# Attention by pairs of heads, with tiled matmuls, ahead of and inside a two-layer MLP kernel on one core

## The chip, the core and the metric

The kernel runs on one core of a Trainium2 chip. A core has TensorE (PE in the profile), which multiplies from SBUF into PSUM, VectorE (DVE), ScalarE (ACT) and GpSimd (POOL), each with its own instruction queue worked in order, and a sync engine (SP) that issues DMAs. The metric is the device time of one execution in microseconds (us).

## What is computed

A banded attention with four sink keys (2 batches, 8 heads, 768 positions, head size 64), then a squared-ReLU MLP, then an MLP with a rational activation, both 512 to 2048 to 512 over 1536 tokens, all in fp32:

```python
scores = scale * np.matmul(q, k.transpose(0, 1, 3, 2))
keep = is_sink | in_window            # n_sink = 4, window = 128
scores = np.where(keep, scores, -1000000000.0)
a = np.exp(scores - np.max(scores, axis=-1, keepdims=True))
a = a / (np.sum(a, axis=-1, keepdims=True) + 1e-09)
x = np.matmul(a, v)                   # to (1536, 512)
h = np.maximum(x @ w_in, 0.0)
x = h * h @ w_out
h = x @ w_in2
g = (a0 + a1*h + a2*h**2 + a3*h**3) / (1 + |b0| |h| + |b1| h**2 + 1e-6)
return g @ w_out2
```

## The kernel before

The 1536 tokens form 12 query tiles of 128 (`TILES`), three to a block (`QT`), four blocks (`BLOCKS`). Queries of tile i look at the keys of their own and the previous tile and at 32 sink columns (`SINK_CAP`), so a head's scores are 128 x 288 (`BAND`), 128 x 128 in the first tile of a batch and 128 x 256 in its second.

**Attention** goes head by head. A *unit* u is one head of one query tile, 96 in all (`U_ALL`). In a slot s each engine does its part of several units: TensorE scores unit s (`score`, L1196 or L1200), turns the probabilities of unit s-2 (`turn_p`, L1216, L1218 for the sinks of four heads at once) and weighs the values for unit s-3 (`weigh`, L1233, L1240 for sinks). VectorE adds the mask and takes the row's minimum of the negated scores (L925), ScalarE takes the exponential with its row sum (L656); the turned probabilities are copied from PSUM to `bpT` by VectorE for even units (L935) and by ScalarE for odd ones (L647). In the first 32 units (`k < EARLY`) a score is one fp32 matmul; TensorE works an fp32 matmul as two records in the trace. Later ones are two fp32r matmuls (L1200, one record each), for which GpSimd splits queries and keys into a high and a low part (`split_kq`, L468 to L488); the input is packed with each head's 64 features twice, so that the contraction is over 128 rows. In `weigh` the turned probabilities are the stationary operand (128 x 128) and 64 columns of values move; the output has queries on rows. After a tile's eighth head VectorE divides by the row sums (`finish`, L941 to L949, into `o_sb`), TensorE transposes the result (`tile_out`, L1259), and ScalarE and VectorE write it as a high and a low part into `xT` (L672, L966).

**The lead.** The first 30 slots (`LEAD`) run with nothing else on TensorE. Scores and turned probabilities have a bank each, and in the lead a second of each (`score_bank`, `turn_bank`): `s_ps` for even units, `y_ps` for odd ones. So `score(u)` waits only until VectorE has read the scores of unit u-2.

**The steady part.** The other slots lie inside the first MLP (layer 1). Per step i a block needs `first` (L1146, 12 matmuls of 384 columns) and `second1` (L1158, 12 more); a list (`events`) puts one slot or tile output after each half of 12 matmuls: after the second group of three in `first` and after the second in `second1`. Between them ScalarE and VectorE square the hidden values (L594, L842, L599, L848). Blocks 0 to 2 carry attention this way; block 3 and the second MLP (L1384 and on) carry none.

## Time and profile before

| | us |
|---|---|
| median of 3 runs | 672.12 (670.58 to 672.66) |
| profiled execution, its own time | 672.72 |
| its span, first to last instruction | 670.9 |
| lead: first score matmul to the first matmul of layer 1 | 7.70 to 44.52 |
| layer 1 with attention inside | 44.52 to 320.32 |
| rest of layer 1 | 320.32 to about 392 |
| second MLP | about 392 to 670.9 |

| engine | busy us | share of the span |
|---|---|---|
| PE | 654.5 | 98% |
| PEld (weight load, overlaps PE) | 617.3 | 92% |
| DVE | 447.9 | 67% |
| ACT | 377.7 | 56% |
| POOL | 330.9 | 49% |

The records of matmuls overlap: each lasts longer than the distance to the next. What a matmul costs in a stream is the distance between starts, read from the timeline, and its record's length beyond that is the time until its result is there.

### The profile page before, as it was taken

The numbers are of one execution on the slowest core, as the hardware profiler recorded it, in microseconds if no ns is written. First come the engines' busy times: TensorE is split into PE (matmuls) and PEld (weight loads), VectorE is DVE, ScalarE is ACT, GpSimd is POOL, SyncE is SP. The second block draws the span as 40 slices with busy tenths as digits, with TensorE's granted clock in tenths as the row PEclk, the third lists the DMA queues.
The fourth block names the chain that finished last, engine by engine and source line by source line (L and its number), as shares of the span: only waits on it lengthen the run. The fifth ranks groups of instructions, "written<-read, shape, count | busy, mean of one in ns | idle before, by whom it ended". The sixth has DMA issues, their size and how long they took to land.

```text
span 670.9 us, 10181 instructions
## 1 busy us (share of the span) xinstructions
PE 654.5 (98%) x3714; PEld 617.3 (92%) x3714; DVE 447.9 (67%) x665; ACT 377.7 (56%) x804; POOL 330.9 (49%) x316
## 2 busy tenths in 40 slices
PE   7999999999999999999999998999999999999997
PEld 6889998999999999999999997889899999999995
DVE  6656564444344344343466679999899989998995
ACT  3755555334444354443322256677877787778874
POOL 3968573313242212300022337777777767776773
PEclk9999999999999999999999999999999999999999
DMA  7743241203311113100043430002100210001001
GB/s 248 258 146 119 97 162 40 64 1 121 93 40 40 40 40 134 40 9 1 20 125 124 127 110 0 1 1 95 48 1 0 95 48 0 1 1 48 1 0 53
DMA packets 28971, 43.49 MB, mean 65 GB/s; under 512 B 4080, under 2 KB 19440, under 8 KB 28400
## 3 DMA queue, kind: packets, MB, share of 16 engines
q1 hardware_dynamic: 28912, 42.74, 19.6%
q8 instruction: 32, 0.52, 0.3%
...
## 4 chain that ended last, share of the span: by engine, by line
PE 77%; DVE 14%; ACT 3%; issue 3%; POOL 2%; DMA 1%; DVEq 0%; SPq 0%; ACTq 0%; POOLq 0%
PE h_ps L1146 22%; PE y_ps L1158 18%; PE y_ps L1384 15%; PE s_ps L1146 7%; PE o_ps L1233 4%; PE o_ps L1146 3%; DVE s_ps L879 3%; PE s_ps L1216 2%; PE s_ps L1200 2%; DVE o_ps L879 2%; DVE sq L842 2%; DVE p_buf L882 1%; DVE p_buf L873 1%; DVE h_ps L879 1%; DMA y_scratch<-xT 1%
## 5 line engine op out<-in xcount | busy, mean ns | idle before, releaser
L1146 PE MATMUL h_ps<-xT,weights 128*128 128x384 f32 x960 | 190.2, 340 | 0.7 <-ACT sq L594 0.7
L1146 PEld LDWEIGHTS h_ps<-xT,weights 128*128 128x128 f32 x960 | 167.4, 188 | 2.5 <-issue 1.0
L1158 PE MATMUL y_ps<-hid,weights 128*128 128x384 f32 x768 | 156.7, 344 | 0.0
L1384 PE MATMUL y_ps<-weights,hid 128*128 128x512 f32 x576 | 144.3, 395 | 2.3 <-POOL hid L561 1.0
L1158 PEld LDWEIGHTS y_ps<-hid,weights 128*128 128x128 f32 x768 | 134.5, 188 | 0.7 <-issue 0.2
L1384 PEld LDWEIGHTS y_ps<-weights,hid 128*128 128x128 f32 x576 | 107.2, 188 | 24.3 <-POOL hid L561 2.4
L656 ACT ACTIVATE bprobs<-bnegs,neg_max 128x288 f32<-128x288 f32 (+2 forms) x96 | 72.0, 759 | 67.2 <-DVE neg_max L925 66.8
L842 DVE TENSOR_TENSOR sq<-sq 128x384 f32<-128x384 f32 x64 | 45.4, 710 | 88.9 <-ACT sq L594 88.8
L561 POOL TENSOR_TENSOR hid<-p_buf,hid 128x384 fp32r<-128x384 f32 x63 | 64.8, 1028 | 40.0 <-ACT hid L762 39.6
L552 POOL TENSOR_TENSOR q_buf<-h_abs,q_buf 128x384 f32<-128x384 f32 x64 | 64.8, 1013 | 34.5 <-ACT q_buf L617 32.0
L879 DVE RECIPROCAL s_ps<-q_buf 128x384 f32<-128x384 f32 x31 | 79.4, 2561 | 3.2
L848 DVE TENSOR_TENSOR hid<-sq,hid 128x384 fp32r<-128x384 f32 x64 | 53.4, 835 | 37.8 <-ACT hid L599 37.8
L482 POOL TENSOR_SCALAR bq_hi<-q_raw 128x512 fp32r<-128x512 f32 x16 | 10.7, 668 | 136.6 <-DMA q_raw<-in_q_pack 115.2
L458 POOL TENSOR_SCALAR weights<-weights_raw 128x1024 fp32r<-128x1024 f32 x24 | 26.2, 1092 | 104.3 <-DMA weights_raw<-in_w_pack 104.1
L594 ACT ACTIVATE sq<-h_ps 128x384 f32<-128x384 f32 x64 | 31.4, 491 | 74.6 <-PE h_ps L1146 74.6
L1146 PE MATMUL s_ps<-xT,weights 128*128 128x384 f32 x384 | 72.5, 337 | 0.0
L1146 PEld LDWEIGHTS s_ps<-xT,weights 128*128 128x128 f32 x384 | 68.3, 188 | 2.5
L556 POOL TENSOR_TENSOR p_buf<-p_buf,h_sb 128x384 f32<-128x384 f32 x64 | 65.3, 1020 | 0.0
L599 ACT ACTIVATE hid<-sq 128x384 fp32r<-128x384 f32 x64 | 33.6, 524 | 51.4 <-DVE sq L842 51.4
L925 DVE CUSTOM_DVE_ANT_0 bnegs<-s_ps,band_bias 128x288 f32<-128x288 f32 (+2 forms) x81 | 34.3, 423 | 36.2 <-PE s_ps L1200 30.3
L762 ACT ACTIVATE hid<-p_buf 128x384 fp32r<-128x384 f32 x63 | 33.0, 524 | 28.9 <-DVE p_buf L882 27.6
L617 ACT ACTIVATE q_buf<-h_abs,abs_b 128x384 f32<-128x384 f32 x64 | 45.4, 709 | 2.1
...
## 6 DMA issues: line engine op xcount, KB each, us to landing
...
```

The costliest lines, as they stand in the source:

```text
L552: pool.tensor_tensor(q_buf[:, i % RING, :], h_abs[:, i % RING, :], q_buf[:, i % RING, :], ALU.mult).then_inc(qmul_ready, 1)
L556: pool.tensor_tensor(p_buf[:, i % RING, :], p_buf[:, i % RING, :], h_sb[:, i % RING, :], ALU.mult).then_inc(pmul_ready, 1)
L561: pool.tensor_tensor(hid2[:, i % RING, LO, :], p_buf[:, i % RING, :], hid2[:, i % RING, HI, :].bitcast(F32), ALU.subtract).then_inc(hid_re ...
L617: nc.scalar.activation(q_buf[:, i % RING, :], h_abs[:, i % RING, :], ACT.Identity, scale=abs_b[:, 1:2], bias=abs_b[:, 0:1]).then_inc(lin_r ...
L656: nc.scalar.activation(bprobs[:, u // GROUP % 2, cols, m % GROUP], bnegs[:, u % N_RING, cols], ACT.Exp, scale=-1.0, bias=neg_max[:, m:m + ...
L842: nc.vector.tensor_tensor(sq[:, i % 2, :], sq[:, i % 2, :], sq[:, i % 2, :], ALU.mult).then_inc(act1_ready, 1)
L848: nc.vector.tensor_tensor(hid[:, i % 2, LO, :], sq[:, i % 2, :], hid[:, i % 2, HI, :].bitcast(F32), ALU.subtract).then_inc(hid_ready, 1)
L879: nc.vector.reciprocal(h_banks[r], q_buf[:, r, :]).then_inc(qinv_ready, 1)
L925: nc.vector.tensor_tensor_reduce(out=bnegs[:, u % N_RING, cols], in0=score_bank(u)[:, cols], in1=band_bias[:, kind, cols], scale=-SCALE, s ...
L1146: ins = nc.tensor.matmul(bank, weights[:, i, wp, W_IN, t * P:(t + 1) * P], x, start=(t == 0 and n == 0), stop=(t == KC - 1 and n == 2))
L1158: ins = nc.tensor.matmul(y_ps[:, m, 0:NT], weights[:, i, wp, W_OUT, m * P:(m + 1) * P], hid[:, i % 2, gp, :], start=(i == 0 and n == 0), s ...
L1384: ins = nc.tensor.matmul(y_bank(turn, t), hid2[:, i % RING, gp, t * P:(t + 1) * P], weights[:, i, wp, W_OUT, :], start=(i == 0 and n == 0) ...
```

## The change

Heads are worked in pairs. A pair p is heads 2c and 2c+1 of a query tile, 48 in all (`P_ALL`); `LEAD` is 15 pairs.

- **Scores.** Inputs are packed with two heads' features on rows 0 to 63 and 64 to 127. Each head's score is one fp32 matmul whose operands lie on 64 rows, one head above the other, into two banks. This holds for all pairs; the fp32r form and GpSimd's splits of queries and keys are gone.
- **Weighing.** 64 columns of values are stationary and 128 turned probabilities move; the two heads write rows 0 to 63 and 64 to 127 of the same bank, so features lie on rows. For sinks there are two matmuls of 128 moving columns in place of one of 256.
- **Division.** The reciprocal row sums are spread over 512 columns (`sums`), transposed on TensorE (`turn_inv`), copied by ScalarE (`inv_copy`) and multiplied by VectorE (`divide`); the transpose of the output goes. VectorE also packs the sinks of four heads (`pack_sinks`).
- **Banks.** One pair of banks (`pair_bank`) holds a pair's scores and then its turned probabilities. In the lead there is a second set for odd pairs. `score(p)` waits for both copies of pair p-2.
- **Order.** A step "A" scores pair p and weighs pair p-2; a step "B" turns pair p-1. In "B" ScalarE takes the second exponential of pair p and then copies for pair p-1. "M" divides, "X" and "L" write the high and low part, "F" turns the reciprocals. In the steady part "A", "B" and "F" take the places that slots had.

```diff
-    U_ALL = H * TILES
-    LEAD = 30
-    EARLY = 8
+    P_ALL = PAIRS * TILES
+    LEAD = 15
...
-        q_raw3 = sb("q_raw3", [P, 3, GROUP * P], F32, band)
-        bk_raw = sb("bk_raw", [P, H, BAND], F32, band)
-
-        bkT = sb("bkT", [P, H, BAND], F32R, band)
-        bq_hi = sb("bq_hi", [P, 2, GROUP * P], F32R, band)
-        bq_lo = sb("bq_lo", [P, 2, GROUP * P], F32R, band)
+        bq = sb("bq", [P, 3, 2 * P], F32, band)
+
+        bk = sb("bk", [P, PAIRS, BAND], F32, band)
...
-        bprobs = sb("bprobs", [P, 2, BAND, GROUP], F32, band)
-        bpT = sb("bpT", [P, P_RING, 3 * P], F32, band)
+        bprobs = sb("bprobs", [P, 2, GROUP, BAND], F32, band)
+        bsinks = sb("bsinks", [P, 2, GROUP, SINK_CAP], F32, band)
+        bpT = sb("bpT", [P, P_RING, 2, 3 * P], F32, band)
...
+        inv_rows = sb("inv_rows", [P, H, D], F32, band)
+        inv_cols = sb("inv_cols", [P, DM], F32, band)
+        x_sb = sb("x_sb", [P, DM], F32, band)
...
+        def pair_bank(p, hp):
+            return y_ps[:, hp, :] if p < LEAD and p % 2 else s_ps[:, hp, :]
+
+        def wait_turned_copies(eng, p):
+
+            eng.wait_ge(pT_by_dve, p + 1)
+            eng.wait_ge(pT_by_act, p + 1)
...
+        def steps(first, last):
+
+
             found = []
-            for s in range(first, slots_before(QT * (blk + 2) - 1) + 1):
-                found += [(s, None)] + [(None, qt) for qt in turned_at(s)]
+            for p in range(first, last):
+                qt = p // PAIRS - 1
+                found.append(("A", p))
+                if p % PAIRS == 1 and qt >= 0:
+                    found.append(("M", qt))
+                    found.append(("X", qt))
+                    if qt >= QT and qt % QT == QT - 1:
+                        found.append(("L", qt))
+                if p <= P_ALL:
+                    found.append(("B", p))
+                if p % PAIRS == 1 and qt >= 0 and not (qt >= QT and qt % QT == QT - 1):
+                    found.append(("L", qt))
+                if p % PAIRS == 0 and qt >= 0:
+                    found.append(("F", qt))
             return found
 
+        def halves_of(blk):
+
+            found = steps(LEAD, P_ALL + 2)
+            ends = [found.index(("L", QT * (b + 2) - 1)) + 1 for b in range(BLOCKS - 1)]
+            halves, e = [[] for _ in range(2 * FT)], -1
+            for kind, n in found[ends[blk - 1] if blk else 0:ends[blk]]:
+                if kind in "ABF" or (kind == "L" and n % QT == QT - 1):
+                    e += 1
+                half = e + e // 14
+                if kind == "X":
+                    half = e + 1 + (e + 1) // 14
+                halves[half].append((kind, n))
+            return halves
+
         def events(blk, i, half):
-
-            found = events_of(blk)
-            return [found[e] for e in range(len(found)) if e + e // 14 == 2 * i + half]
+            return halves_of(blk)[2 * i + half]
...
             def load_k(k):
 
-                if EARLY + 2 <= k:
-                    sp.wait_ge(kq_ready, k - EARLY - 1)
-                elif 4 <= k:
-                    sp.wait_ge(u_scored, GROUP * (k - 1))
-                sp.dma_start(bk_raw[:, heads_of(k), own_cols(k)], k_pack[k]).then_inc(k_loaded[k % 4], 16)
+                if 4 <= k:
+                    sp.wait_ge(p_scored, 2 * (k - 1))
+                sp.dma_start(bk[:, 2 * (k % 2):2 * (k % 2) + 2, own_cols(k)],
+                             k_pack[k].rearrange("p (c n) -> p c n", c=2)).then_inc(k_loaded[k % 4], 16)
...
-            def split_k(heads, cols, done):
-
-                pool.tensor_scalar(bkT[:, heads, cols], bk_raw[:, heads, cols], 1.0, 0.0, ALU.mult, ALU.add
-                                   ).then_inc(bk_high, 1)
-                splits[0] += 1
-                pool.wait_ge(bk_high, splits[0])
...
+                def turned_copy(p):
+                    act.wait_ge(pair_turned, p + 1)
+                    if p >= P_RING:
+                        act.wait_ge(p_pv, p - P_RING + 1)
+                    cols = turned_cols(p, 1)
+                    nc.scalar.activation(bpT[:, p % P_RING, 1, 0:cols], pair_bank(p, 1)[:, 0:cols], ACT.Copy
+                                         ).then_inc(pT_by_act, 1)
...
+                def inv_copy(qt):
+                    act.wait_ge(inv_turned, qt + 1)
+                    if qt:
+                        act.wait_ge(o_read, qt)
+                    nc.scalar.activation(inv_cols[:, :], inv_bank(qt), ACT.Copy).then_inc(inv_copied, 1)
...
+                    act.wait_ge(o_read, qt + 1)
                     nc.scalar.activation(xT[:, blk % 2, HI, :, j * P:(j + 1) * P],
-                                         x_bank(qt).rearrange("p (c n) -> p c n", c=KC), ACT.Copy
+                                         x_sb[:, :].rearrange("p (c n) -> p c n", c=KC), ACT.Copy
...
+                    if kind == "A" and n < P_ALL:
+                        exp(2 * n)
+                    if kind == "B":
+                        if n < P_ALL:
+                            exp(2 * n + 1)
+                        if n:
+                            turned_copy(n - 1)
+                    if kind == "F":
+                        inv_copy(n)
+                    if kind == "X":
+                        x_high(n)
...
+                def pack_sinks(g):
+
+                    dve.wait_ge(u_exp, GROUP * (g + 1))
+                    if g >= 2:
+                        dve.wait_ge(pair_turned, 2 * (g - 1))
+                    nc.vector.tensor_copy(bsinks[:, g % 2, :, :], bprobs[:, g % 2, :, 0:SINK_CAP]
+                                          ).then_inc(sinks_packed, 1)
...
+                        dve.wait_ge(inv_turned, qt)
+                    nc.vector.tensor_copy(inv_rows[:, :, :], row_inv[:, :].rearrange("p (h o) -> p h o", o=1
+                                          ).to_broadcast([P, H, D])).then_inc(inv_spread, 1)
+
+                def divide(qt):
+
+                    dve.wait_ge(inv_copied, qt + 1)
+                    dve.wait_ge(p_pv, PAIRS * (qt + 1))
+                    if qt:
+                        dve.wait_ge(tile_ready, qt)
+                    nc.vector.tensor_tensor(x_sb[:, :], o_bank(qt), inv_cols[:, :], ALU.mult).then_inc(o_read, 1)
...
+                def score(p):
+                    qt, c, i = pair(p)
+                    k = p // 2
+                    if c % 2 == 0:
+                        pe.wait_ge(k_loaded[k % 4], 16 * (k // 4 + 1))
+                        pe.wait_ge(q_loaded[k % 3], 16 * (k // 3 + 1))
+                    if i == 2 and c == 0:
...
+                    if p >= 2:
+                        wait_turned_copies(pe, p - 2)
+                    if p == LEAD:
+                        pe.wait_ge(u_negs, 2 * p)
+                    if p > LEAD and c == 1:
+                        pe.wait_ge(inv_copied, qt)
...
+                    for hp in range(2):
+                        rows = slice(D * hp, D * hp + D)
+                        ins = nc.tensor.matmul(pair_bank(p, hp)[:, cols], bq[rows, k % 3, P * (c % 2):P * (c % 2) + P],
+                                               bk[rows, c, cols], start=True, stop=True)
+                    ins.then_inc(p_scored, 1)
+
+                def turn_p(p):
+                    qt, c, i = pair(p)
+                    g = p // 2
+                    pe.wait_ge(u_exp, 2 * p + 2)
+                    if LEAD <= p + 1 < P_ALL:
+                        pe.wait_ge(u_negs, 2 * p + 4)
+                    for hp in range(2):
+                        for t in range(1 if i == 0 else 2):
+                            keys = slice(SINK_CAP + t * P, SINK_CAP + (t + 1) * P)
+                            ins = nc.tensor.transpose(pair_bank(p, hp)[:, t * P:(t + 1) * P],
+                                                      bprobs[:, g % 2, 2 * (c % 2) + hp, keys], ident[:, :])
+                    if with_sinks(p):
+
+                        pe.wait_ge(sinks_packed, qt // KT * 2 * (KT - 2) + 2 * (i - 2) + c // 2 + 1)
+                        ins = nc.tensor.transpose(pair_bank(p, 1)[:, 2 * P:3 * P],
+                                                  bsinks[:, g % 2, :, :].rearrange("p h n -> p (h n)"), ident[:, :])
+                    ins.then_inc(pair_turned, 1)
...
+                def weigh(p):
+                    qt, c, i = pair(p)
+                    k, r = p // 2, p % P_RING
+                    wait_turned_copies(pe, p)
...
-                        ins = nc.tensor.matmul(bank[:, D * m:D * (m + 1)], bpT[:, u % P_RING, t * P:(t + 1) * P],
-                                               bv[:, t, D * m:D * (m + 1)], start=(m == 0 and t == 0),
-                                               stop=(m == H - 1 and t == last), skip_group_check=True)
...
+                    tiles = 1 if i == 0 else 2
+                    for t in range(tiles):
+                        for hp in range(2):
+                            at = D * (2 * c + hp)
+                            ins = nc.tensor.matmul(bank[D * hp:D * hp + D, c * P:(c + 1) * P],
+                                                   bv[:, t, at:at + D], bpT[:, r, hp, t * P:(t + 1) * P],
+                                                   start=(c == 0 and t == 0),
+                                                   stop=(i < 2 and c == KC - 1 and t == tiles - 1),
+                                                   skip_group_check=True)
...
+                        for cc in (c - 1, c):
+                            ins = nc.tensor.matmul(bank[:, cc * P:(cc + 1) * P], bvs[:, cc * P:(cc + 1) * P],
+                                                   bpT[:, r, 1, 2 * P:3 * P], start=False, stop=(cc == KC - 1),
+                                                   skip_group_check=True)
...
+                def turn_inv(qt):
+                    pe.wait_ge(inv_spread, qt + 1)
...
+                def step(kind, n):
+                    if kind == "A":
+                        if n < P_ALL:
+                            score(n)
+                        if n >= 2:
+                            weigh(n - 2)
+                    if kind == "B" and n:
+                        turn_p(n - 1)
+                    if kind == "F":
```

On TensorE in the lead, from query tile 2 on: before (L1196 is a score, L1216 a turn, L1233 a weighing):

```order
L1196 MATMUL s_ps<-bk_raw,q_raw 128x288
L1216 MATMUL s_ps<-ident,bprobs 128x128 x2
L1233 MATMUL o_ps<-bv,bpT 128x64 x2
L1196 MATMUL y_ps<-bk_raw,q_raw 128x288
L1216 MATMUL y_ps<-ident,bprobs 128x128 x2
```

and after (L1158 is now a pair's scores, L1193 the weighing, L1171 the turn):

```order
L1158 MATMUL s_ps<-bk,bq 128x288 x2
L1193 MATMUL y_ps<-bpT,bv 64x128 x4
L1171 MATMUL y_ps<-ident,bprobs 128x128 x4
L1176 MATMUL y_ps<-ident,bsinks 128x128
L1158 MATMUL y_ps<-bk,bq 128x288 x2
```

Two units of three short groups became one pair of three longer ones, and the weighing now stands ahead of the turn.

On ScalarE at the same place in the lead: before (L656 is an exponential, L647 a copy of turned probabilities):

```order
L656 ACTIVATE bprobs,row_sum<-bnegs,neg_max 128x288
L647 ACTIVATE bpT<-y_ps 128x256
L656 ACTIVATE bprobs,row_sum<-bnegs,neg_max 128x288 x2
L647 ACTIVATE bpT<-y_ps 128x256
L656 ACTIVATE bprobs,row_sum<-bnegs,neg_max 128x288 x2
```

and after (L596 is an exponential, L605 a copy, L612 the copy of the reciprocals, L619 the high part):

```order
L605 ACTIVATE bpT<-s_ps 128x256
L596 ACTIVATE bprobs,row_sum<-bnegs,neg_max 128x288 x2
L605 ACTIVATE bpT<-y_ps 128x384
L612 ACTIVATE inv_cols<-y_ps 128x512
L596 ACTIVATE bprobs,row_sum<-bnegs,neg_max 128x288
L619 ACTIVATE xT<-x_sb 128x4x128
L596 ACTIVATE bprobs,row_sum<-bnegs,neg_max 128x288
```

The counts are the same, two exponentials to a copy, but the copy behind the two exponentials of pair p is that of pair p-1, whose banks the scores of pair p+1 need.

On TensorE in the steady part: before (L1158 and L1146 are layer 1, L1200 the fp32r scores):

```order
L1158 MATMUL y_ps<-hid,weights 128x384 x6
L1146 MATMUL h_ps<-xT,weights 128x384 x6
L1200 MATMUL s_ps<-bkT,bq_hi 128x288
L1200 MATMUL s_ps<-bkT,bq_lo 128x288
L1216 MATMUL s_ps<-ident,bprobs 128x128 x2
L1233 MATMUL o_ps<-bv,bpT 128x64 x2
```

and after (L1122 and L1110 are layer 1 now):

```order
L1110 MATMUL h_ps<-xT,weights 128x384 x6
L1158 MATMUL s_ps<-bk,bq 128x288 x2
L1193 MATMUL o_ps<-bpT,bv 64x128 x4
L1110 MATMUL h_ps<-xT,weights 128x384 x6
L1122 MATMUL y_ps<-hid,weights 128x384 x6
L1171 MATMUL s_ps<-ident,bprobs 128x128 x4
```

Every second place between the halves of layer 1 now holds a pair's scores and weighing, the other a pair's turn.

## Rows read from the trace of the kernel before

**Rows 1.** The page: busy us, share of the span, instructions

```profile
PE 654.5 (98%) x3714; PEld 617.3 (92%) x3714; DVE 447.9 (67%) x665; ACT 377.7 (56%) x804; POOL 330.9 (49%) x316
```

**Rows 2.** Lead and steady part: length, busy us of PE, PEld, DVE, ACT, POOL, clock, DMA

```profile
7.70:44.52 36.82, 33.56 (x220) 28.82 (x219) 25.29 (x94) 25.01 (x75) 26.42 (x18) 1.00 0.78 251
44.52:320.32 275.80, 271.44 (x1715) 267.43 (x1715) 127.92 (x304) 124.27 (x288) 92.30 (x80) 1.00 0.20 65
```

**Rows 3.** Timeline of TensorE in the lead: start, length, line, count of records

```profile
25.64 0.70 PE L1196 MATMUL y_ps<-bk_raw,q_raw 128*128 128x288 f32 x2
26.18 0.39 PE L1216 MATMUL y_ps<-ident,bprobs 128*128 128x128 f32 x2
26.41 0.56 PE L1233 MATMUL o_ps<-bv,bpT 128*128 128x64 f32 x4
26.81 0.70 PE L1196 MATMUL s_ps<-bk_raw,q_raw 128*128 128x288 f32 x2
...
34.05 0.65 PE L1240 MATMUL y_ps<-bvs,bpT 128*128 128x256 f32 x2
34.54 0.65 PE L1196 MATMUL y_ps<-bk_raw,q_raw 128*128 128x288 f32 x2
```

**Rows 4.** Timeline of TensorE, narrow scores early in the lead

```profile
12.45 0.44 PE L1196 MATMUL y_ps<-bk_raw,q_raw 128*128 128x128 f32 x2
12.72 0.28 PE L1216 MATMUL y_ps<-ident,bprobs 128*128 128x128 f32 x1
```

**Rows 5.** Timelines of ScalarE and VectorE in the lead

```profile
8.58 0.52 ACT L656 ACTIVATE bprobs<-bnegs,neg_max 128x128 f32<-128x128 f32 x1 [4.84 <-DVE neg_max L925]
8.98 0.51 ACT L656 ACTIVATE bprobs<-bnegs,neg_max 128x128 f32<-128x128 f32 x1
31.17 0.82 ACT L656 ACTIVATE bprobs<-bnegs,neg_max 128x288 f32<-128x288 f32 x1 [1.85 <-DVE neg_max L925]
31.84 0.83 ACT L656 ACTIVATE bprobs<-bnegs,neg_max 128x288 f32<-128x288 f32 x1
34.91 0.82 ACT L656 ACTIVATE bprobs<-bnegs,neg_max 128x288 f32<-128x288 f32 x1
35.66 0.38 ACT L647 ACTIVATE bpT<-y_ps 128x256 f32<-128x256 f32 x1
```

**Rows 6.** All engines in the lead: from a score to its exponential

```profile
26.39 0.46 DVE L925 CUSTOM_DVE_ANT_0 bnegs<-y_ps,band_bias 128x288 f32<-128x288 f32 x1 [0.36 <-PE y_ps L1196]
...
26.89 0.83 ACT L656 ACTIVATE bprobs<-bnegs,neg_max 128x288 f32<-128x288 f32 x1
```

**Rows 7.** Lead: the division, the masks; ScalarE's high part by form

```profile
30.07 0.69 DVE L949 TENSOR_TENSOR o_sb<-o_ps,row_inv 128x512 f32<-128x512 f32 x1
...
12.71 2.03 DVE L889 TENSOR_SCALAR band_bias<-sq 128x32 bf16<-128x32 f32 x3
...
L672 ACT ACTIVATE xT<-s_ps 128x512 fp32r<-128x512 f32 x9 | 5.3, 586 | 6.6 <-DMA y_scratch<-xT 4.5 <-PE s_ps L1259 2.2
```

**Rows 8.** Timeline of TensorE in the steady part, each the start of a layer-1 half

```profile
304.01 1.20 PE L1146 MATMUL h_ps<-xT,weights 128*128 128x384 f32 x6
...
307.04 1.22 PE L1158 MATMUL y_ps<-hid,weights 128*128 128x384 f32 x6
...
309.83 1.21 PE L1146 MATMUL h_ps<-xT,weights 128*128 128x384 f32 x6
```

**Rows 9.** Timeline of TensorE in layer 1 without attention

```profile
322.40 2.28 PE L1158 MATMUL y_ps<-hid,weights 128*128 128x384 f32 x12
...
326.60 2.28 PE L1158 MATMUL y_ps<-hid,weights 128*128 128x384 f32 x12
```

**Rows 10.** Steady part by form: busy us, mean ns, idle before; then L1216 (min/median/max)

```profile
L1158 PE MATMUL y_ps<-hid,weights 128*128 128x384 f32 x552 | 115.7, 346 | 0.0
L1233 PE MATMUL o_ps<-bv,bpT 128*128 128x64 f32 x262 | 37.1, 261 | 0.3 <-DVE o_sb L949 0.3
...
L1216 PE MATMUL s_ps<-ident,bprobs x152: 270/280/385, 9.2 to 311.0; 128*128 128x128 f32 x152
```

366 lines of the change are left out of this document (104 added, 262 removed).

## The prediction

> **What bounds the kernel now.** The first view is the page's busy times: TensorE is busy for 654.5 of 670.9 us, 98% [rows 1], so the change has to be costed on it first. The second is the table of stretches [rows 2]. Attention lies in the first two: the lead, 36.82 us, in which TensorE is busy for 33.56, and the steady part, 275.80 us, in which it is busy for 271.44 and idle for 4.36. The granted clock is 1.00 (2.4 GHz) in both. The third is TensorE's timeline, where the cost of a group is the distance from its start to the next one's. In the lead a unit takes 26.81 - 25.64 = 1.17 us: the score 0.54, the turn 0.23, the weighing 0.40 [rows 3]. In the steady part a layer-1 step without attention takes 326.60 - 322.40 = 4.20 us for 24 matmuls, 0.175 each [rows 9]. The stretch 304.01 to 307.04 holds 12 of these and one whole unit, so the unit costs 3.03 - 2.10 = 0.93; the next, 307.04 to 309.83, lacks the score, so turn and weighing cost 0.69 and the score 0.24 [rows 8]. No other engine works in these stretches for even half of the time except in the lead, where ScalarE has 25.01 and VectorE 25.29 of 36.82 us [rows 2]. The lead is therefore the place where a longer chain through them would show.
>
> **The lead becomes a serial loop.** Before, score(u) waits only for VectorE's reading of the scores of u-2, and TensorE streams. Now score(p+1) waits for both copies of pair p-1, since it shares their banks. ScalarE's copy for p-1 stands behind both exponentials of pair p, and these need score(p). So nothing overlaps on the path: score, mask and minimum, two exponentials, copy, score. For 288 columns:
> - copy 0.38, from 35.66 [rows 5]
> - handing over, 0.05: VectorE starts at 26.39, 0.05 behind the end of the score that began at 25.64 and lasted 0.70 [rows 3, 6]
> - a weight load that isn't ahead of its matmul, 0.10: a turn's matmul lasts 280 ns in the median and 385 at most [rows 10]
> - the two heads' scores. One lasts 0.70 with a distance of 0.54, that is two records of 0.27 and 0.16 of tail [rows 3]. For two heads, four records: 0.70 if they run side by side throughout, 1.24 one after the other. the timeline shows the records starting in the order of the program, and here head 1's first record is queued behind head 0's second. Then only the middle two overlap: 3 x 0.27 + 0.16 = 0.97. I take this value; no row here shows matmuls on half the rows, and the other two are the ends
> - 0.05 again, VectorE 0.46, and 0.04 to ScalarE at 26.89 [rows 6]
> - exponentials: 0.67 from one to the next (31.17, 31.84) and 0.75 to a copy (34.91, 35.66) [rows 5]
>
> The sum is 3.47 us a pair, 3.20 and 3.74 at the ends, where two units took 2.34. TensorE's own work, about 2, hides in it. For 128 columns the score's distance is 0.27, 0.135 a record [rows 4], and exponentials follow by 0.40 [rows 5]: about 2.25. For 256 I take 3.2, near the wide form.
>
> score(2) can start at about 10.6: the first score at 7.7, four exponentials from 8.6 at 0.40 [rows 5], and a copy. Then 2 turns of 2.25, and 0.65 more where the masks, 2.03 us on VectorE [rows 7], outlast a turn: 5.2. Four turns of 3.2: 12.8. Six of 3.47: 20.8. The three tile ends each add two things. The sums and the turned reciprocals are on VectorE and then TensorE ahead of the next score, late by some 0.2. Then the division, 0.69, and ScalarE's high part, 0.59 [rows 7], stand between two exponentials, and delay the second by some 0.8. Together 3.0. The last pair's score, mask and turn ahead of layer 1: 2.4. The lead ends at 10.6 + 5.2 + 12.8 + 20.8 + 3.0 + 2.4 = 54.8 instead of 44.52, **+10.2**; with the ends, +7.2 and +13.2. It leaves as much for the steady part as before: 30 heads scored, 28 turned.
>
> **Steady part, TensorE's work.** 33 pairs are scored here, 25 of 288 columns, 4 of 256, 4 of 128.
> - Scores: before 33 x 0.48 = 15.8. Now three distances a pair: 25 x 0.81 + 4 x 0.73 + 4 x 0.40 = 24.8, **+9.0**. Side by side throughout it would be two distances, +0.7, one after the other four, +17.2.
> - Weighing: before 262 records [rows 10] at 0.40 / 4 = 0.0975 (0.39 to 0.40 a unit) [rows 3], 25.5. Now 128 columns move where 64 did, but half of the columns of the array are used by each head. A record is 0.12 by the 0.27 of 288 columns, and 0.135 by the narrow score [rows 3, 4]; I take 0.12. A pair has 8 records and, overlapped by one as above, 5 distances: 31 pairs with 5 and 4 with 3 make 167 x 0.12 = 20.0, **-5.5**. Throughout side by side 132 x 0.12: -9.7. In turn 264 x 0.12: +6.2.
> - The sinks' matmul of 256 columns took 0.49 [rows 3]; now four records of 0.12: **0**. Turns are the same, and four transposes of reciprocals stand where four of outputs did: 0.
> - Going over from one layout of the array to another, three times a pair: into 64 rows, into 64 columns, and back to the whole. No row shows it. The lower end is 0. The upper is a full drain and a load that isn't ahead: 0.346 - 0.175 = 0.17 of tail, and 0.10 [rows 9, 10], 0.27 in all, 27 us. I take 0.10, the row that shows an engine restarted with no weights loaded: 100 x 0.10 = **+10**.
>
> The Trainium skill ("TensorEngine Tiling (Array Packing)", Key Properties) states that changing the tiling mode, not just the tile, drains TensorE. That speaks for the upper end, by which the sum would be 17 us higher; no trace of the kernel before can show it.
>
> **Waits in the steady part.** "B" now waits until both scores of pair p are read. Between "A" and "B" lie 12 matmuls, 2.1 us, and VectorE needs 2 x 0.46 behind the score's end. In front of it may stand one hidden step of layer 1; I estimate that it still comes out about 0.5 before "B". Both copies of p-1 come behind that step too, some 0.3 before the next "A". A tile end uses this up, with 0.59 more on ScalarE. I put 2 us on these in place of 4.4 [rows 2]: **-2.4**. GpSimd's splits of queries and keys were under other work and give nothing; block 3 and the second MLP are untouched.
>
> Sum: 672.7 + 10.2 + 9.0 - 5.5 + 10 - 2.4 = **694**. The profiled execution, 672.7, is 0.6 above the median of 672.1, less than the uncertainty of any term, so the forecast for the median is 694 too.
>
> **Rivals.**
> - *Fully side by side.* If both heads start together, lead +7.2, scores +0.7, weighing -9.7, changes of layout +10, waits -2.4: 678.5. For it speaks that the halves share no rows or no columns; against it that fp32 makes two records of each matmul and TensorE starts them in order. The Trainium skill ("TensorE: Matmul & The Clock Gate", Part 3) gives about 4 ns between the starts of matmuls on different tiles. By that rule this case holds; whether it does for fp32's two records no row here shows.
> - *Not side by side at all*: the change doesn't do what its layout says. Lead +13.2, scores +17.2, weighing +6.2, layouts +10, waits -2.4: 717.
> - *Faster.* Fully side by side, and a change of layout and an unloaded restart cost nothing: lead +5.9, scores +0.7, weighing -9.7, waits -2.4: 667. One mechanism decides it, weights for the next layout loading under the last matmuls of the one before. With scores and weighing fully overlapped it pays below about 0.05 us a change.
>
> **How the numbers follow.** Forecast 0.42, fully side by side 0.26, not at all 0.14, faster 0.12; 0.06 for ends about level. Another 17 us for drains is within the range on top of the forecast's lower variants, not of the serial case. The range from 668 to 716 leaves out about half of the fastest case and the serial case with dear changes. A measurement of this kernel can tell about 0.3% from no change. Faster 0.12, same 0.06, slower 0.82.
>
> **What the profile after would show.** The lead ending near 55 with TensorE idle for a third of it, ScalarE's copies directly followed by the next pair's score, and exponentials idle about 1.7 us a pair. In the timeline the start of head 1's first record beside head 0's second, 0.27 behind head 0's first; at the same time, and it is the second case; 0.54 behind it, the third. Between a pair's weighing and the next layer-1 matmul, 0.1 more than a plain distance. In block 0 to 2 a step of 4.2 us plus about 2.3 a pair. I am wrong if the lead isn't longer, or if a pair costs TensorE less than the 1.86 of two units.

## The result and the profile after

The changed kernel takes 698.55 us (median of 4 runs, 696.34 to 700.63); the kernel before took 671.84 beside it. The ratio is 1.0399, with a 95% interval of 1.0363 to 1.0435. The profiled execution took 698.31 us. The page of the kernel after, its head and the busy times, which answer to [rows 1]:

```profile
span 696.4 us, 10235 instructions
PE 660.4 (95%) x3746; PEld 588.7 (85%) x3746; DVE 443.3 (64%) x693; ACT 369.5 (53%) x816; POOL 257.6 (37%) x242
```

TensorE is busy for 660.4 us, 5.9 more than before, but the span is 25.5 us longer. One instant splits the span well: the first matmul of layer 1, where the lead ends. Before it stood at 44.52, so the rest took 626.4 us. Now it stands at 59.63, the rest takes 636.8. **The lead is 15.1 us longer and the rest 10.4.**

**The lead.** Windows of the kernel after (the columns are those of [rows 2]: length, busy time of each engine with its instructions, granted clock, DMA share, GB/s):

```profile
7.83:14.98 7.15, 2.38 (x22) 1.48 (x21) 5.61 (x18) 2.85 (x14) 4.36 (x3) 0.82 1.03 321
14.98:39.90 24.92, 19.13 (x89) 11.17 (x89) 11.83 (x43) 9.42 (x32) 12.67 (x8) 0.50 0.33 106
39.90:59.63 19.73, 13.71 (x113) 8.72 (x112) 13.01 (x39) 10.49 (x32) 10.19 (x6) 1.00 0.48 131
```

Before, the granted clock was 1.00 all through the lead [rows 2]. Now TensorE has gaps of 1.21 and 2.96 us at the start, and then runs 24.9 us at 0.50, the 1.2 GHz level. In the longer gap VectorE makes the masks that the next scores need, while GpSimd subtracts from 10.87 to 13.21:

```profile
10.95 2.48 DVE L841 TENSOR_SCALAR band_bias<-sq 128x128 bf16<-128x128 f32 x2
```

The timeline in the part at full clock shows the loop (start, duration, group; in brackets the idle time ahead of it and what ended it):

```profile
43.74 0.76 PE L1158 MATMUL s_ps<-bk,bq 64*128 64x288 f32 x4 [1.91 <-ACT bpT L605]
44.43 0.66 PE L1193 MATMUL y_ps<-bpT,bv 128*64 128x128 f32 x8
45.02 0.66 PE L1171 MATMUL y_ps<-ident,bprobs 128*128 128x128 f32 x4
...
46.09 0.47 ACT L605 ACTIVATE bpT<-y_ps 128x384 f32<-128x384 f32 x1
46.70 0.76 PE L1158 MATMUL y_ps<-bk,bq 64*128 64x288 f32 x4 [0.80 <-ACT bpT L605]
...
49.84 0.76 PE L1158 MATMUL s_ps<-bk,bq 64*128 64x288 f32 x4 [0.72 <-DVE bpT L896]
```

L1158 is the scores, L1193 the weighing, L1171 the turn, L605 and L896 the copies. A pair takes 2.96 and 3.14 us. The scores follow the copies, as the prediction said, but a copy needs two things: ScalarE free of its exponentials, and the turn done. Here both come almost together, the turn's last record at 45.90 and ScalarE's copy at 46.09. At half clock, for pairs of 256 columns, the distances are 27.93 to 31.81 and 31.81 to 35.85, 3.88 and 4.04 us, and the turn comes last:

```profile
27.93 1.22 PE L1158 MATMUL s_ps<-bk,bq 64*128 64x256 f32 x4 [1.33 <-ACT bpT L605]
29.08 1.12 PE L1193 MATMUL o_ps<-bpT,bv 128*64 128x128 f32 x8
30.13 1.12 PE L1171 MATMUL y_ps<-ident,bprobs 128*128 128x128 f32 x4
30.16 0.49 ACT L596 ACTIVATE bprobs<-bnegs,neg_max 128x256 f32<-128x256 f32 x1
31.28 0.39 ACT L605 ACTIVATE bpT<-y_ps 128x256 f32<-128x256 f32 x1 [0.54 <-PE y_ps L1171]
31.81 1.22 PE L1158 MATMUL y_ps<-bk,bq 64*128 64x256 f32 x4 [0.57 <-DVE bpT L896]
```

ScalarE is done with its exponentials at 30.65 and then waits 0.54 us for the turn. So here TensorE's own scores, weighing and turn are the loop, with only a copy between.

**TensorE's work in the steady part.** The four score records of a pair (two heads, two records each) take 0.76 us in all, and the next group starts 0.69 behind their start. Windows on L1158 alone show how they lie:

```profile
322.30:322.45 0.15, 0.09 (x2) 0.10 (x2) 1.00 0.00 0
322.62:322.78 0.16, 0.16 (x4) 0.04 (x2) 1.00 0.00 0
```

Two records are under way in the first 0.09 us, all four 0.3 us later. The two heads' first records start 7 ns apart. Both heads run side by side from the start. Timeline of a steady pair with its surroundings:

```profile
284.72 0.60 PE L1171 MATMUL s_ps<-ident,bprobs 128*128 128x128 f32 x4
285.07 1.30 PE L1122 MATMUL y_ps<-hid,weights 128*128 128x384 f32 x6
...
297.23 1.21 PE L1110 MATMUL h_ps<-xT,weights 128*128 128x384 f32 x6
298.36 0.76 PE L1158 MATMUL s_ps<-bk,bq 64*128 64x288 f32 x4
299.05 0.66 PE L1193 MATMUL o_ps<-bpT,bv 128*64 128x128 f32 x8
299.64 0.60 PE L1202 MATMUL o_ps<-bpT,bvs 128*128 128x128 f32 x3
```

Scores take 0.69 and weighing 0.59, each with its change of layout; six layer-1 matmuls ahead of the scores take 1.13. The turn takes 0.35.

**The waits.** From 60 us to the end of attention TensorE has three long waits, 3.43, 3.26 and 3.17 us, all for ScalarE's copy. The timeline of all engines around the first and second:

```profile
112.98 0.43 SPq L328 DMA_DIRECT2D weights_raw<-in_w_pack  x1
116.91 1.06 ACT L587 ACTIVATE weights<-weights_raw 128x1024 fp32r<-128x1024 f32 x1 [4.97 <-DMA weights_raw<-in_w_pack]
118.91 0.36 ACT L605 ACTIVATE bpT<-s_ps 128x256 f32<-128x256 f32 x1
119.42 1.33 PE L1158 MATMUL s_ps<-bk,bq 64*128 64x288 f32 x4 [3.43 <-ACT bpT L605]
120.68 1.12 PE L1193 MATMUL o_ps<-bpT,bv 128*64 128x128 f32 x8
121.73 2.29 PE L1122 MATMUL y_ps<-hid,weights 128*128 128x384 f32 x6
...
184.94 0.35 SPq L358 DMA_DIRECT2D y_scratch<-xT  x1
190.68 0.63 ACT L619 ACTIVATE xT<-x_sb 128x512 fp32r<-128x512 f32 x1 [3.65 <-DMA y_scratch<-xT]
191.71 0.36 ACT L605 ACTIVATE bpT<-s_ps 128x256 f32<-128x256 f32 x1
192.22 0.70 PE L1158 MATMUL s_ps<-bk,bq 64*128 64x256 f32 x4 [3.26 <-ACT bpT L605]
```

ScalarE stands 4.97 us before weights that SyncE issued only at 112.98, and 3.65 us before a store issued at 184.94. SyncE issues in order, and a load of values that waits for weighing (issued at 111.38 and 184.16) stood ahead of both. ScalarE's copy is queued behind, and TensorE's next scores wait for it. After the wait the clock is down: six L1122 matmuls take 2.09 us at 121.73, twice their usual 1.05.

### The profile page after: what moved, and what is told of

It is laid out like the page before. It is cut to its first block, busy times and chain, and to the rows that moved or that the text cites. A ratio compares the mean times of both kernels' runs of the same rounds, so it can differ in the third digit from the quotient of the medians.

```text
span 696.4 us, 10235 instructions
## 1 busy us (share of the span) xinstructions
PE 660.4 (95%) x3746; PEld 588.7 (85%) x3746; DVE 443.3 (64%) x693; ACT 369.5 (53%) x816; POOL 257.6 (37%) x242
## 4 chain that ended last, share of the span: by engine, by line
PE 80%; DVE 11%; issue 2%; DMA 2%; ACT 2%; POOL 2%; SPq 0%; DVEq 0%; ACTq 0%; POOLq 0%
PE h_ps L1110 23%; PE y_ps L1122 19%; PE y_ps L1342 14%; PE s_ps L1110 7%; PE s_ps L1158 4%; PE o_ps L1193 3%; PE o_ps L1110 3%; DVE s_ps L831 3%; PE s_ps L1171 2%; DVE o_ps L831 2%; DMA y_scratch<-xT 2%; DVE p_buf L834 1%; PE o_ps L1202 1%; DVE p_buf L825 1%; DVE h_ps L831 1%
## 5 line engine op out<-in xcount | busy, mean ns | idle before, releaser
L1110 PE MATMUL h_ps<-xT,weights 128*128 128x384 f32 x960 | 192.3, 342 | 0.7 <-ACT sq L542 0.7
L1110 PEld LDWEIGHTS h_ps<-xT,weights 128*128 128x128 f32 x960 | 169.0, 190 | 4.1 <-issue 2.8
L1122 PE MATMUL y_ps<-hid,weights 128*128 128x384 f32 x768 | 157.9, 346 | 0.0
L1122 PEld LDWEIGHTS y_ps<-hid,weights 128*128 128x128 f32 x768 | 136.0, 191 | 2.0 <-issue 2.0
L794 DVE TENSOR_TENSOR sq<-sq 128x384 f32<-128x384 f32 x64 | 36.3, 568 | 87.0 <-ACT sq L542 86.9
L596 ACT ACTIVATE bprobs<-bnegs,neg_max 128x288 f32<-128x288 f32 (+2 forms) x96 | 48.2, 502 | 77.8 <-DVE neg_max L878 77.8
L1110 PE MATMUL s_ps<-xT,weights 128*128 128x384 f32 x384 | 72.4, 337 | 0.0
L1110 PEld LDWEIGHTS s_ps<-xT,weights 128*128 128x128 f32 x384 | 68.3, 188 | 2.5
L800 DVE TENSOR_TENSOR hid<-sq,hid 128x384 fp32r<-128x384 f32 x64 | 46.0, 719 | 37.8 <-ACT hid L547 37.8
L474 POOL TENSOR_TENSOR weights<-weights_raw,weights 128x1024 fp32r<-128x1024 f32 x16 | 38.0, 2372 | 44.0 <-ACT weights L587 43.3
L878 DVE CUSTOM_DVE_ANT_0 bnegs<-s_ps,band_bias 128x288 f32<-128x288 f32 (+2 forms) x82 | 31.8, 424 | 32.8 <-PE s_ps L1158 31.2
L1158 PE MATMUL s_ps<-bk,bq 64*128 64x288 f32 (+2 forms) x164 | 31.3, 459 | 17.7 <-ACT bpT L605 15.6
```

Of the source, the lines that this page charges most:

```text
L474: pool.tensor_tensor(weights[:, i, LO, :, :], weights_raw[i][:, LO, :], weights[:, i, HI, :, :].bitcast(F32), ALU.subtract).then_inc(w_rea ...
L596: nc.scalar.activation(bprobs[:, u // GROUP % 2, m % GROUP, cols], bnegs[:, u % N_RING, cols], ACT.Exp, scale=-1.0, bias=neg_max[:, m:m + ...
L794: nc.vector.tensor_tensor(sq[:, i % 2, :], sq[:, i % 2, :], sq[:, i % 2, :], ALU.mult).then_inc(act1_ready, 1)
L800: nc.vector.tensor_tensor(hid[:, i % 2, LO, :], sq[:, i % 2, :], hid[:, i % 2, HI, :].bitcast(F32), ALU.subtract).then_inc(hid_ready, 1)
L1110: ins = nc.tensor.matmul(bank, weights[:, i, wp, W_IN, t * P:(t + 1) * P], x, start=(t == 0 and n == 0), stop=(t == KC - 1 and n == 2))
L1122: ins = nc.tensor.matmul(y_ps[:, m, 0:NT], weights[:, i, wp, W_OUT, m * P:(m + 1) * P], hid[:, i % 2, gp, :], start=(i == 0 and n == 0), s ...
```

## Experiments

All were timed beside the kernel before, in several batches; it took 671.84 us beside the kernel after and 672.8 to 673.1 in the others, so times from different batches compare to about 1 us, and ratios are the safer guide. "Lead end" is the first layer-1 matmul of the profiled execution, "rest" is its span less that. Both are of one execution: the kernel after and e3 have the same code up to there, and their leads end 1.7 us apart.

| kernel | us | ratio | lead end | rest |
|---|---|---|---|---|
| before | 671.84 | 1 | 44.52 | 626.4 |
| after | 698.55 | 1.040 | 59.63 | 636.8 |
| e1 copy first | 696.61 | 1.034 | 57.96 | 636.6 |
| e2 clock filler | 695.00 | 1.033 | 57.19 | 634.7 |
| e3 loads early | 682.69 | 1.013 | 61.35 | 621.0 |
| e4 same rows | 731.05 | 1.085 | 73.42 | 655.5 |
| e5 whole rows | 711.19 | 1.056 | 64.06 | 645.8 |
| e6 whole columns | 708.38 | 1.053 | 60.93 | 646.9 |
| e8 turn first | 686.63 | 1.020 | 61.63 | 624.4 |
| e9 turn first, filler | 685.97 | 1.020 | 61.59 | 621.1 |
| e10 before, loads early | 671.08 | 0.999 | 44.61 | 623.3 |
| e11 lead order | 680.07 | 1.013 | 56.58 | 621.2 |
| e12 lead order, filler | 679.48 | 1.010 | 57.97 | 621.0 |
| e13 GpSimd later | 677.20 | 1.006 | 47.51 | 628.4 |

**Side by side or not.** `e4` puts both heads' scores on rows 0 to 63 (the second head's scores aren't computed):

```diff
-                        rows = slice(D * hp, D * hp + D)
+                        rows = slice(0, D)
```

> The changed kernel, but the score matmuls of both heads take rows 0 to 63, so the second head's scores are those of the first (this part of the result is not computed). Overlap theory: in the changed kernel the two heads' matmuls run side by side in halves of the rows; on the same rows they must follow each other, 2 more distances of 0.27 us a pair: 33 x 0.54 = 17.8 us in the steady part, and 0.54 in each turn of the lead's loop, 7 us; together 20 to 27 us slower than the changed kernel, with score to next start 1.2 instead of 0.68. Rival (no overlap, the matmuls on 64 rows are simply shorter): no difference.

It took 32.5 us more, over the range. `e5` takes `slice(0, P)` instead, the whole array:

> Both heads' scores are computed on all 128 rows of the array, one matmul behind the other, instead of each on its 64 rows; each result is then the sum of both heads' scores, so the heads' own scores are not computed. Beside the run with both heads on rows 0 to 63 (731.05 us, serial too) this takes away nothing but the row layout: a pair changes the array's layout twice (before and behind weighing) instead of three times. Theory (a change costs about 0.10 us, and the pairing of row halves, not the layout, was what the earlier run lost): about 3.3 us less over the 33 steady pairs and 1 us less in the lead, so 726 to 728 us, with the four score records still about 1.2 us. Rival (a change of layout costs a record's distance, 0.27 us): 9 to 11 us less, 720 to 722 us. Rival (changes are free): 730 to 732 us.

The first theory gave 726 to 728; it measured 711.2. Timelines of the two at a steady pair, e4 first:

```profile
284.55 1.22 PE L1122 MATMUL y_ps<-hid,weights 128*128 128x384 f32 x6
285.69 1.23 PE L1158 MATMUL s_ps<-bk,bq 64*128 64x288 f32 x4
286.86 0.66 PE L1193 MATMUL o_ps<-bpT,bv 128*64 128x128 f32 x8
287.44 1.32 PE L1122 MATMUL y_ps<-hid,weights 128*128 128x384 f32 x6
```

```profile
282.08 1.22 PE L1122 MATMUL y_ps<-hid,weights 128*128 128x384 f32 x6
283.14 1.13 PE L1158 MATMUL s_ps<-bk,bq 128*128 128x288 f32 x4
284.20 0.66 PE L1193 MATMUL o_ps<-bpT,bv 128*64 128x128 f32 x8
284.79 1.33 PE L1122 MATMUL y_ps<-hid,weights 128*128 128x384 f32 x6
```

In e4 the scores take 1.17 where the kernel after takes 0.69. So the halves do save 0.48 us for a pair of 288 columns and less for narrower ones, some 15 us over 33 pairs, of the 18.7 that the rest grew; the others go to the clock (23.1 us of the rest at 0.50 in place of 13.7). From e4 to e5 the two groups become 0.08 (1.14 to 1.06) and 0.11 (1.17 to 1.06) shorter, 0.19 in all, for the one change of layout that the edit takes away. The starts of single records show that both parts belong to the way into the row halves: the first score record starts 0.268 behind the last one of layer 1 (0.176 in e5), the second 0.347 behind the first (0.242), while the way out, from the last score record to the first of weighing, is 0.333 and 0.336. So a change costs nearly twice the 0.10 of the theory, and less than the 0.27 of its rival. That makes 6 of the 9.7 us in the rest; 9.5 us less of it at half clock, worth up to 4.7, covers the others. As much again, 9.4 us, is in the lead, which neither case of the expectation had. Its windows from 15 us to the lead's end, e4 and then e5, tell why:

```profile
15.00:65.00 50.00, 42.52 (x158) 26.72 (x159) 17.51 (x69) 16.37 (x53) 19.54 (x12) 0.50 0.31 93
```

```profile
15.00:64.06 49.06, 37.46 (x200) 24.40 (x200) 22.97 (x79) 20.19 (x65) 23.21 (x14) 0.78 0.38 113
```

e4 spent 50 us at half clock, e5 less than half of its time. A comparison of totals would have put this on the layout.

**The weighing.** `e6` weighs with 128 stationary columns, so both heads write the whole bank one after the other (the outputs of single heads aren't computed):

```diff
-                            ins = nc.tensor.matmul(bank[D * hp:D * hp + D, c * P:(c + 1) * P],
-                                                   bv[:, t, at:at + D], bpT[:, r, hp, t * P:(t + 1) * P],
+                            ins = nc.tensor.matmul(bank[:, c * P:(c + 1) * P],
+                                                   bv[:, t, at:at + 2 * D], bpT[:, r, hp, t * P:(t + 1) * P],
```

> Both heads' values are weighed with 128 stationary columns, so each head's eight matmuls write the whole bank one behind the other; the bank then holds sums over the wrong values, and the outputs of single heads are not computed. Scores stay on halves of the rows. Theory (the two heads' weighing runs side by side in halves of the columns: eight records in 0.59 us with one layout change): serial they take 8 x 0.12 = 0.96 and one change of layout (0.10) goes, so +0.27 to +0.37 us a pair and +9 to +12 us over the 33 steady pairs; the lead, which waits on the copies, moves by under 2 us: 707 to 713 us against 698.6 for the changed kernel. Rival (the weighing was serial all along, and the records' ends only overlap): no more than the change of layout, 695 to 699 us.

708.4 is within the range, and its rest grew by 10.1 us. In the timeline of e6 the weighing takes 0.92 from its start to the next group's, where the kernel after takes 0.59:

```profile
316.77 0.76 PE L1158 MATMUL s_ps<-bk,bq 64*128 64x288 f32 x4
317.45 1.16 PE L1193 MATMUL o_ps<-bpT,bv 128*128 128x128 f32 x8
318.37 1.30 PE L1122 MATMUL y_ps<-hid,weights 128*128 128x384 f32 x6
```

So both halves of the change do on TensorE what they say.

**The late loads.** `e3` issues three weight tiles a round in place of two, and each store ahead of the load of values:

```diff
-                    elif 2 * k - 9 < FT:
-                        for i in range(2 * k - 9, min(2 * k - 7, FT)):
+                    elif 3 * k - 18 < FT:
+                        for i in range(3 * k - 18, min(3 * k - 15, FT)):
                             load_weights(0, i)
-                    load_v(k)
-                    if k == 13:
-                        load_sinks(1)
                     if k == 15:
                         store_y(0)
                     if k == 21:
                         store_y(1)
+                    load_v(k)
+                    if k == 13:
+                        load_sinks(1)
```

> The changed kernel with only the sync engine's order changed: the last seven weight loads of layer 1 are issued one to two key loads earlier, and the two stores of layer-1 results ahead of the value load of their round instead of behind it. Theory: the three TensorE waits of 3.2 to 3.4 us in the steady part (at 119, 192 and 290 us) come from ScalarE waiting for weights 15 (4.97 us) and for the two stores (7.2 us), with the copy for the next scores behind it; all three go, 9 to 10 us, a further 1 to 2 us with the clock that falls after them. Rival (the bank dependence of scores on copies makes these waits in itself, the DMA only happens to be last): less than 3 us.

The time fell by 15.9 us (the ratio from 1.040 to 1.013), and in the profiled executions all of that is in the rest (636.8 to 621.0). The three waits are gone, 9.9 us. The other 6 are the clock: in ten-microsecond windows the kernel after has a granted clock of 0.91 and 0.75 from 110 to 130 us and 0.83 from 190 and from 290, which loses 6.8 us, 0.6 of them while TensorE still waited, and e3 has 1.00 from its lead's end on. `e10` makes the same edit in the kernel before:

> The kernel before with the same earlier issue of the weights and the two stores that took 15.9 us out of the changed kernel. Theory (the late weights and stores cost the kernel before next to nothing, since its copies stood behind them without TensorE waiting: 1.45 us of waits there): the time falls by 0 to 3 us, to 670 to 673 us, and the changed kernel with early loads (682.7) stays 10 to 13 us behind it, about what its longer lead costs. Rival (the loads hold the kernel before up as much, hidden in many small waits): it falls by over 5 us, to 667 or less.

It changed nothing that can be told (0.9988, 0.9964 to 1.0012). The late loads were there all along; they cost only once ScalarE's copy stood between them and TensorE. With them out of both kernels, the rest of the changed kernel is no longer than that of the kernel before (621.0 against 623.3, single executions), and **all of the remaining loss is in the lead**, 61.35 against 44.61.

**The lead: order and clock.** `e1` puts, in the lead, ScalarE's copy for pair p-1 ahead of the second exponential of pair p:

```diff
                     if kind == "B":
+                        if 0 < n < LEAD:
+                            turned_copy(n - 1)
                         if n < P_ALL:
                             exp(2 * n + 1)
-                        if n:
+                        if n >= LEAD:
                             turned_copy(n - 1)
```

> The changed kernel with one edit: in the lead ScalarE copies the turned probabilities of pair p-1 ahead of the second exponential of pair p, not behind it. Serial-loop theory: score(p+1) waits for that copy, so the loop is cut by the second exponential (0.54 us at the end of the lead) and the lead, 7.8 to 59.6 us, ends 6 to 15 us earlier, more where TensorE, busier, keeps its clock. Rival (the lead is long because TensorE itself takes longer for a pair, or because of VectorE's masks and tile ends): the copy was not on the path, and the lead moves by less than 2 us.

`e2` queues two fp32 matmuls of 256 columns, with unused results, behind each turn of the lead:

> The changed kernel with two more fp32 matmuls of 256 columns (identity by identity, into a bank that nothing reads) behind each turn in the lead, 13 times, in the time in which TensorE waits for copies. Clock theory: the granted clock of 0.50 between 15 and 40 us comes from a half-idle TensorE and stretches each pair's score from about 0.76 to 1.33 us and each transposition of reciprocals; with the filler the clock stays near 1.00 and the lead ends 3 to 6 us earlier although more work is done. Rival (the low clock is only a companion, the loop runs through ScalarE and VectorE): same time within 1 us, or later by the filler's own 0.9 us a pair where it outlasts the wait.

e1 gave 1.9 us, with the lead's end 1.7 earlier: no more than two executions of the same lead differ, and the case of its rival (under 2). That fits the timeline above, where the turn ends only 0.19 ahead of ScalarE's copy, so that the copy could not start much earlier. e2 gave 3.6, though it adds work, 2.4 of them in the lead, short of its theory's 3 to 6; in the rest it has half clock behind only one of the three waits (1.00 from 110 to 130 and from 280 to 300 us), which is worth more than the 2.1 us that its rest is shorter. The granted clock from 15 us to the lead's end was 0.92 in e2, 0.77 in e1 and 0.72 in the kernel after. `e8` joins e1 and e3 and turns pair p-1 ahead of weighing pair p-2; `e9` adds one filler matmul behind each weighing of e8:

```diff
+                    if kind == "B" and 2 <= n < LEAD:
+                        weigh(n - 2)
```

> Three edits of order together: ScalarE takes the copy of pair p-1 ahead of pair p's second exponential in the lead (696.6 alone), the weights and the two stores are issued earlier (682.7 alone), and in the lead TensorE turns pair p-1 ahead of weighing pair p-2, so that the copies start 0.6 us earlier. Theory (the lead is a loop scores, exponentials, turn, copies, next scores, and each link taken out of it shortens a pair by its duration): copy ahead of the exponential and turn ahead of weighing take 0.7 and 0.6 us out of a pair's 3.1 at full clock, for 15 pairs; with some of it at half clock or taken by the next wait, the lead ends at 42 to 50 us instead of 61.4 in the run with the early loads, and the time is 667 to 676 us. Rival (VectorE and GpSimd's masks bound the lead beside the loop): the lead ends at 54 to 58, 678 to 681 us. Rival (the slower steady part decides): no less than 680.

> The run with the three edits of order, and behind each weighing of the lead one fp32 matmul of 256 columns more, whose result is not used. Theory (the granted clock falls to 0.50 where TensorE idles much in the lead, and this filler keeps it up): the half-clock stretch shrinks by 5 us or more, the time is 1 to 4 us under the run without the filler. Rival (with the turn ahead of weighing TensorE is dense enough already): the filler only stands in the way, 0 to 3 us slower.

Both missed: 686.6 is above e3's 682.7, with a lead as long and half clock on to 70.0 us, 8.4 us into the rest; and the filler raised the clock from 0.72 to 0.82 and moved the lead's end by 0.04 us. With the turn out of the way, other things stood ahead of the copies. `e11` puts the copies first, on ScalarE ahead of both exponentials and on VectorE ahead of the sums, the division and the low part:

> The run with the turn ahead of weighing (686.6 us), and in the lead alone four more moves: ScalarE takes the copy of pair p-1 ahead of both exponentials of pair p (except where the sinks are packed), VectorE takes its copy ahead of the row sums, of the division and of the low part, and the turn of the reciprocals stands behind the next pair's scores. Theory (what stood ahead of the copies was the loop: in the run before, TensorE waited 1.88 and 1.86 us for ScalarE's copy behind a division and a high part, 0.55 to 3.6 us for the reciprocals): 1.9 us a tile from the copies and up to 1 us a tile from the reciprocals go, and 0.7 us a pair where the loop closes over ScalarE; the lead ends at 42 to 50 us instead of 61.6, and the time is 668 to 677 us. Rival (half clock stretches whatever is left, and GpSimd's work stretches VectorE's): the lead ends at 52 to 58, 679 to 684 us.

> The run with all edits of order in the lead, and one fp32 matmul of 256 columns behind each weighing of the lead, whose result is not used. In the last pair of runs such a filler shortened the half-clock stretches and moved the time by 0.7 us. Theory (the lead is bound by the copies and exponentials, not by TensorE's clock): within 2 us of the run without the filler. Rival (at half clock TensorE's own work is in the loop): 3 to 8 us faster than it.

The theory missed here as well (lead end 56.6, 680.1 us), and the filler again gave nothing. The timeline of e11 around its longest wait shows what held it:

```profile
44.95 2.34 POOL L483 TENSOR_TENSOR weights<-weights_raw,weights 128x1024 fp32r<-128x1024 f32 x1
...
45.04 2.34 DVE L901 COPY bsinks<-bprobs 128x128 f32<-128x128 f32 x1
...
47.43 0.48 PE L1191 MATMUL y_ps<-ident,bsinks 128*128 128x128 f32 x1 [2.62 <-DVE bsinks L901]
```

A copy that took 0.22 us elsewhere lasted until GpSimd's subtraction ended, and so did the addition of 1e-9 to the row sums (128x8) at the first tile's end:

```profile
18.83 2.35 POOL L483 TENSOR_TENSOR weights<-weights_raw,weights 128x1024 fp32r<-128x1024 f32 x1
...
18.95 2.25 DVE L915 TENSOR_SCALAR row_den<-row_sum 128x8 f32<-128x8 f32 x1
```

`e13` therefore holds GpSimd's weights 2 to 7 back until the lead's last scores are out:

```diff
                 for i in range(EARLY_W):
+                    if i == 2:
+                        pool.wait_ge(p_scored, LEAD)
                     weight_high(0, i)
                     weight_low(i)
```

> The run with all edits of order in the lead (680.07 us), and GpSimd rounds weights 2 to 7 only once the lead's last scores are out; ScalarE's high parts of weights 8 to 15 stand three steps later to match. Theory (VectorE's instructions whose operands lie in SBUF alone stand still while GpSimd subtracts two SBUF operands: in the run without this edit a 128x8 sum took 2.25 us instead of 0.16 and ended with GpSimd's at 21.2, a 128x128 copy 2.34 instead of 0.22, a low part 2.03 instead of 0.69, and each stood ahead of a copy that TensorE waited for): VectorE's busy time in the lead falls by 5 us or more, no such instruction takes over 1 us behind 18 us, 4 to 8 us of the lead go, and the time is 672 to 676 us, level with the kernel before (672.8). Rival (the copies and exponentials bound the lead on their own): the lead ends at 54 us or later, 678 to 681 us. Rival (GpSimd's work behind the lead now meets VectorE's there and the weights come late): waits of TensorE for weights behind the lead, no gain or a loss.

ScalarE's high parts of weights 8 to 15 stand three steps later to match. The lead ends at 47.51, 9.1 us earlier, VectorE's busy time in it falls from 33.7 to 27.2, and the addition on 128x8 takes 0.16. But the time is 677.2, 1.2 over the range, because part of the third case came true too. Its rest is 7.2 us longer. Behind the lead GpSimd now meets VectorE's layer-1 work, and TensorE waits. The timeline of e13 there:

```profile
62.10 2.40 POOL L483 TENSOR_TENSOR weights<-weights_raw,weights 128x1024 fp32r<-128x1024 f32 x1
62.32 2.46 DVE L924 COPY inv_rows<-row_inv 128x512 f32<-128x512 f32 x1
...
65.77 2.52 POOL L483 TENSOR_TENSOR weights<-weights_raw,weights 128x1024 fp32r<-128x1024 f32 x1
...
66.68 2.03 DVE L815 TENSOR_TENSOR hid<-sq,hid 128x384 fp32r<-128x384 f32 x1 [0.59 <-ACT hid L558]
68.63 0.41 DVE L911 COPY bpT<-s_ps 128x256 f32<-128x256 f32 x1
69.30 1.09 PE L1231 MATMUL s_ps<-ident,inv_rows 128*128 128x128 f32 x4 [3.65 <-DVE bpT L911]
```

With the wait of 0.95 at 59.33 and the clock of 0.90 and 0.76 in the two windows from 60 to 80 us, 3.4 us of work, this covers the 7.2. No version here beats the kernel before (e13: 1.0061, 1.0039 to 1.0083).

## Why the forecast held, and where it didn't

The forecast of 694 was 4.6 us low, and it was composed of terms of which several failed. That it came so close is luck: errors of about the same size stood on both sides.

- **The lead.** That the next scores wait for both copies is as told. At full clock a pair takes 2.96 to 3.14, under the 3.20 that the prediction set as its low end: side by side the scores take 0.69, and the exponentials follow each other by 0.53 where the sum had 0.67. The step that failed is "TensorE's own work, about 2, hides in it". At full clock it just about does; at 0.50 it doesn't, and scores, weighing, turn and copy make 3.88 and 4.04 where the sum had 3.2. The granted clock stood in no term: durations were taken at 1.00 for a TensorE that was made to wait a third of the time. Stretch by stretch, scores 2 to 4 took 6.8 us where the sum had 5.2, the four pairs of 256 columns with one tile end (17.60 to 35.85) 18.3 for 13.8, and the six of 288 with two (35.85 to 57.41) 21.6 for 22.8. So all of the excess, 15.1 us instead of 10.2 and beyond the upper end of 13.2, lies where the clock was mostly 0.50.
- **VectorE in the lead.** In the same stretch VectorE stood under GpSimd's subtractions. The masks took 2.48 us (0.36 in e13) with TensorE waiting 2.96, and the addition on 128x8 at 20.08 took 1.26 (0.16 in e13) on the way to the reciprocals, for which TensorE waited 2.60. The sum had 0.65 for the masks and 0.2 for the reciprocals. It has no term for the low part. Before, that one reads its first operand from PSUM (`y_ps`) and takes 0.69; the changed one reads both from SBUF (`x_sb`, `xT`), and three of them took 1.51 us in the mean, 2.07 at 56.51 under GpSimd's subtraction. In e13, with GpSimd held back, they took 0.69. How the 4.9 us of excess divide between the clock and this no run shows.
- **Scores and weighing.** "then only the middle two overlap" was wrong; both heads overlap throughout. A pair's two groups cost 0.69 + 0.59 = 1.28, of which some 0.4 are changes of layout; the sum had 0.81 + 0.60 + 0.20 = 1.61. The rival "fully side by side" had this mechanism, as the rule cited there from the Trainium skill ("TensorE: Matmul & The Clock Gate", Part 3) had it: the trace agrees, with the two heads' first records 7 ns apart, where the Trainium skill gives 4.
- **Changes of layout.** 0.10 each was too little. Into the row halves a change costs 0.19. From rows or the whole array into column halves it's 0.09 ahead of the first record and 0.05 behind it, and back to the whole 0.10 and 0.10 (0.202 to the first layer-1 record where 0.102 is a plain distance, then 0.28 in place of 0.175). That is some 0.5 a pair where the sum had 0.30. The drain of 0.27 wasn't seen. The Trainium skill's rule that a new tiling mode drains TensorE ("TensorEngine Tiling (Array Packing)", Key Properties) may hold, but it costs no full tail here. Two errors offset each other in part: the records run more side by side than the sum had it, and the changes are dearer.
- **Waits in the steady part.** "I put 2 us on these in place of 4.4" is the step that failed most. There were 9.9 us in three waits, and 6 more at half clock behind them. The prediction moved ScalarE's copy behind the exponentials and asked only what VectorE and layer 1 do there. The rows of before had late stores and loads on ScalarE's queue, and I never asked who would now stand behind them.

The sum can be set against what TensorE's records show. "Measured" adds up, in the rest, the distances from each record's start to the next without the waits, for e3 less e10, both at full clock there:

| term | forecast | measured |
|---|---|---|
| lead | +10.2 | +15.1 |
| scores, weighing, changes of layout | +13.5 | +1.1 (+3.4, -4.1, and +1.8 in layer 1 around them) |
| turns and sinks | 0 | -2.2 (-4.5 and +2.3) |
| waits in the rest, late loads apart | -2.4 | -1.3 |
| late loads, with the clock behind them | none | +15.8 |

The measured terms give 28.5 and the spans 25.5; the rest of e10 is 3.1 shorter than that of before in these single executions. On the rest, errors of 13 to 17 us and of 16 us cancelled: forecast +11.1, and +10.4 measured. "Turns are the same" also failed, by 4.5 us. Of what the profile after was to show, half came. The lead ended near 60, not 55, with TensorE idle for a third (busy 35.2 of 51.8 us); ScalarE's copies are followed by the next scores; head 1 starts with head 0, which it had named as the mark of the second case; and a pair costs TensorE less than the 1.86 of two units (0.69 + 0.59 + 0.35 for a turn = 1.63, and 1.8 with the 0.19 that the changes of layout put on the layer-1 groups around it), which it had named as the mark of being wrong.

What stays open: how much of the lead's 15.1 us the clock alone costs. e2, with its own filler in the loop, ended the lead 2.4 us earlier, little more than the 1.7 between two executions of the same lead. In e9 and e12, with the turn ahead of weighing, more clock gave nothing that can be told. GpSimd was held back only together with all edits of order (e13), not in the kernel after. The exponentials' gain (288 columns: 529 ns in the mean, 818 before) and the turns' (0.12 us a record before, 0.09 in e3) came with probabilities that are written, and read by the turns, contiguously instead of with a stride of four; no run took that apart.
